# Attention set-up: 64 powers scanned and the rest made by ScalarE, chunk 0 scaled behind the reciprocal, a semaphore of its own for the gate, products of zeros first

## The chip, the cores and the metric

The kernel runs on one core of one Trainium2 chip. The metric is the device time of one execution in microseconds (us), here the median of three runs. The core's engines are TensorE (PE, with its weight loads as PEld), VectorE (DVE), ScalarE (ACT), GpSimd (POOL) and SyncE (SP), which issues most of the DMAs.

## The reference

Three stages follow one another. The change touches the set-up of the first one.

```python
# 1. linear attention with decay; B, H, S, D = 4, 8, 768, 48
for t in range(S):
    cur = einsum('bhd,bhe->bhde', u * k[t], v[t])
    y[t] = einsum('bhd,bhde->bhe', r[t], state + cur)
    state = w[:, :, None] * state + einsum('bhd,bhe->bhde', k[t], v[t])
# 2. top-1 mixture of experts on 3072 tokens of 384, 8 experts of 1024
x = gate_w[:, None] * (relu(x @ w1[e]) @ w2[e])        # e = argmax of the logits of a token
# 3. RMS norm and a gated feed-forward layer, 384 -> 1536 -> 384
out = (silu(xn @ w_gate) * (xn @ w_val)) @ w_out
```

## The kernel before

**The attention stage** cuts the 768 steps of each of 4 batches into 6 chunks of 128 (P); heads go in NP = 4 pairs, the two heads of a pair on partitions 0 to 47 and 64 to 111. In a chunk the recurrence becomes matrix products: queries are scaled by powers of the decay w and keys by inverse powers (rkt = rk_in * rk_decay, `scale_rk`, L795), TensorE makes the scores (`scores`, L1078), VectorE copies those below the diagonal into am, which already holds the bonus of u on its diagonal (L826, by the mask causal), and TensorE multiplies am by v (L1116) on top of what the state of the chunk before contributes (L1111). The next state needs kd = k * tail (POOL, L524), multiplied by v (L1103); tail is w raised to the remaining steps of the chunk. A last product turns y over and computes the logits in one go (`turn_x`, L1088, with turn_gate: the identity beside w_gate).

**Queues.** Each engine has its own program, whose instructions start in the order written, and they meet by semaphores. A chunk c (g counts chunks of all batches) is:
- VectorE (`batch`, L816): the two copies into am (L826), the bonus sum of chunk c + 1 (L802, needs POOL's ruk), `scale_rk` of chunk c + 2, the new state (L839), half of the diagonal of chunk c + 1 (L808), the sum of logits (L813). In chunk 2 of the first batch `token_setup` (L775) follows, which prepares what the routing needs.
- ScalarE (`batch`, L628): the decayed state (L635), x of the chunk before (L613, L614), the other half of the diagonal (L622), xt (L603).
- POOL (`batch`, L519): kd (L524), then ru = r * u (L514) and ruk = ru * k (L517) of the next chunk.
- TensorE (`batch`, L1091): scores of chunk c + 1, kd times v, `turn_x` of the chunk before, L1111, L1116.
- SP: load_columns (rk_in, three buffers; a load waits for `rk_scaled`), load_v, load_rows (rkn_in), and the stores of x.

**The set-up ahead of chunk 0.** VectorE scans w into powers 0 to 128 for each pair (L756); copies powers 0 to 63 to the upper half of r_decay (L758) and power 128 to chunk_decay (L759); takes the reciprocal of powers 64 down to 1 into its lower half (L761); copies r_decay in reverse into k_decay (L762); makes tail_t, the products of power 64 with powers 127 down to 0 (L766); then scales chunk 0 (L795); then `later_setup` waits for const_ld (L770), casts the mask to causal (L771), waits for the four memsets of POOL and raises z_ready; then bonus (L802) and half diagonal (L808) of chunk 0, and `scale_rk(0, 1)`. ScalarE issues the loads of u_b, const, turn_gate, bias_b, rms_gain and modality_i (L583 to L588), waits for const_ld, and copies the identity into turn_gate (L590). const_ld counts two loads, const (which holds the identity and the mask) and the gate's part of turn_gate. TensorE waits for const_ld (L1064), turns tail_t over (`decays_by_rows`, L1067), ScalarE copies that to tail (L596), and TensorE does the scores of chunk 0. POOL clears state and kd (L506), makes ru and ruk of chunk 0, and waits for tail before kd.

**Behind attention** the tokens are routed, the experts run in tiles of 256 tokens with weights and activations split in a high and a low part (three products each, L1156), and the feed-forward layer does the same in 6 blocks of 512 tokens.

## Time and profile before

| | |
|---|---|
| median of 3 runs | 861.05 us (860.03 to 861.21) |
| the profiled execution | 858.51 us |
| its span, first to last instruction | 856.7 us |
| mean granted TensorE clock | 0.98 of full |
| busy share of the span | PE 94%, DVE 41%, ACT 33%, POOL 18% |
| chain that ended last, by engine | PE 88%, DVE 6%, issue 2%, DMA 1%, ACT 1% |
| its largest line | L1156 (experts and feed-forward), 78% |
| bytes moved | 63.15 MB, mean 74 GB/s |

The attention stage is the first 139 us. The profile's page says where the whole time goes; of the first microseconds only the timeline, the chain of waits in order of time and the table of loads tell enough. Times in them count from the span's start. A row of the timeline merges equal instructions that follow one another: "x4" with 1.37 us are four instructions in 1.37 us. A matmul of fp32 operands leaves two records, so L1078's 8 matmuls count as 16. "DVEq" and the like are an engine's sequencer, "issue" a stretch in which it waited for nothing that the profile shows. In square brackets stands how long the engine had been idle and what ended that.

### The profile page before, as it was taken

What the parts mean: (1) busy time and instruction counts of PE and PEld (TensorE: products, weight loads), DVE (VectorE), ACT (ScalarE), POOL (GpSimd) and SP (SyncE); (2) the same over time, 40 slices, a digit from 0 to 9 for tenths busy, and PEclk for the clock granted to TensorE, in tenths of its full rate; (3) what the DMA queues carried; (4) which work ended last, traced back from release to release, by engine and by line L of the source; (5) the groups of instructions that cost most, each with busy time, mean ns of one, the idle gap of its engine ahead of it and who ended that gap; (6) DMA issues with size and microseconds to landing.
All of it is one profiled execution on the core that took longest, in us unless ns stands there. A gap on an engine that the chain in (4) does not pass through costs nothing.

```text
span 856.7 us, 14691 instructions
## 1 busy us (share of the span) xinstructions
PE 809.5 (94%) x5219; PEld 743.3 (87%) x5219; DVE 353.0 (41%) x662; ACT 285.6 (33%) x678; POOL 157.8 (18%) x138
## 2 busy tenths in 40 slices
PE   4999994499999999998999999999999999999998
PEld 4898883399999999997889888988988898898888
DVE  8999996643325332234252144024214402420330
ACT  3676672343335343333222123023212212221320
POOL 7787670312222122221000000000000000000000
PEclk9999998599999999999999999999999999999999
DMA  8688861421226222112000100110010001000001
GB/s 251 204 260 246 243 193 47 165 94 64 80 74 218 92 71 76 67 56 71 0 2 19 56 1 0 39 35 0 18 55 0 0 37 37 0 18 19 1 0 38
DMA packets 29034, 63.15 MB, mean 74 GB/s; under 512 B 4786, under 2 KB 17358, under 8 KB 28992
## 3 DMA queue, kind: packets, MB, share of 16 engines
q1 hardware_dynamic: 24224, 52.71, 19.4%
q0 software_dynamic: 3584, 9.46, 3.4%
q10 hardware_dynamic: 1184, 0.45, 0.2%
q8 instruction: 22, 0.36, 0.2%
q14 instruction: 20, 0.16, 0.1%
HBM read 49.62 MB, written 14.56 MB: 75 GB/s over the span
## 4 chain that ended last, share of the span: by engine, by line
PE 88%; DVE 6%; issue 2%; DMA 1%; ACT 1%; POOL 0%; DVEq 0%; ACTq 0%; POOLq 0%
PE bank L1156 78%; PE bank L1078 2%; PE bank L1116 2%; PE bank L1088 2%; PE bank L1103 1%; PE bank L1111 1%; PE bank L1149 1%; DVE am L808 1%; PE bank L1197 1%; DMA turn_gate<-w_gate 1%; DVE rkt L795 1%; DVE am L826 1%; DVE row_hot L915 1%; DVE bonus L802 1%; DVE state L839 1%
## 5 line engine op out<-in xcount | busy, mean ns | idle before, releaser
L1156 PE MATMUL bank<-xn_hi,ffn_hi 128*128 128x512 f32 x432 | 168.9, 391 | 2.9 <-DVE xn_lo L1022 2.9
L1156 PE MATMUL bank<-xn_lo,ffn_hi 128*128 128x512 f32 x432 | 168.7, 391 | 0.0
L1156 PE MATMUL bank<-xn_hi,ffn_lo 128*128 128x512 f32 x432 | 168.6, 390 | 0.0
L1041 DVE TENSOR_TENSOR prod<-silu,bank 128x512 f32<-128x512 f32 x72 | 49.5, 687 | 281.5 <-ACT silu L724 281.5
L724 ACT ACTIVATE silu<-bank 128x512 f32<-128x512 f32 x72 | 43.1, 598 | 221.2 <-PE bank L1156 221.2
L1156 PEld LDWEIGHTS bank<-xn_hi,ffn_hi 128*128 128x128 f32 x432 | 81.5, 189 | 19.9 <-issue 3.1
L1156 PE MATMUL bank<-ffn_hi,hh 128*128 128x384 f32 x288 | 97.1, 337 | 0.0
L1156 PE MATMUL bank<-ffn_hi,hl 128*128 128x384 f32 x288 | 96.3, 335 | 0.0
L1156 PE MATMUL bank<-ffn_lo,hh 128*128 128x384 f32 x288 | 96.3, 334 | 0.0
L1156 PEld LDWEIGHTS bank<-xn_hi,ffn_lo 128*128 128x128 f32 x432 | 81.5, 189 | 17.0
L1156 PEld LDWEIGHTS bank<-xn_lo,ffn_hi 128*128 128x128 f32 x432 | 81.5, 189 | 16.9
L1156 PE MATMUL bank<-xg_hi,w_hi 128*128 128x256 f32 x312 | 89.1, 286 | 2.0 <-DVE xg_lo L930 2.0
L1156 PE MATMUL bank<-xg_lo,w_hi 128*128 128x256 f32 x312 | 88.9, 285 | 0.0
L1156 PE MATMUL bank<-xg_hi,w_lo 128*128 128x256 f32 x312 | 88.9, 285 | 0.0
L968 DVE SCALAR_TENSOR_TENSOR h_lo<-bank,h_hi 128x512 fp32r<-128x512 f32 x52 | 35.9, 691 | 128.4 <-ACT h_hi L685 128.4
L1156 PE MATMUL bank<-w_hi,h_hi 128*128 128x384 f32 x208 | 71.0, 341 | 0.0
L1156 PE MATMUL bank<-w_hi,h_lo 128*128 128x384 f32 x208 | 69.9, 336 | 0.0
L1156 PE MATMUL bank<-w_lo,h_hi 128*128 128x384 f32 x208 | 69.9, 336 | 0.0
L1156 PEld LDWEIGHTS bank<-xg_hi,w_hi 128*128 128x128 f32 x312 | 60.5, 194 | 2.4 <-DVE xg_lo L930 2.4
L1156 PEld LDWEIGHTS bank<-xg_lo,w_hi 128*128 128x128 f32 x312 | 60.5, 194 | 0.0
L1156 PEld LDWEIGHTS bank<-xg_hi,w_lo 128*128 128x128 f32 x312 | 60.4, 194 | 0.0
L685 ACT ACTIVATE h_hi<-bank 128x512 fp32r<-128x512 f32 x52 | 31.1, 597 | 72.8 <-PE bank L1156 72.8
(146 smaller groups left out, 1247.7 us busy)
## 6 DMA issues: line engine op xcount, KB each, us to landing
rk_in<-rk_t SPq DMA_DIRECT2D x24, 448.0 KB, 4.3
rkn_in<-rk_n SPq DMA_DIRECT2D x24, 384.0 KB, 4.7
ffn_raw<-ffn_w SPq DMA_DIRECT2D x12, 576.0 KB, 3.7
w_raw<-w SPq DMA_DIRECT2D x16, 384.0 KB, 4.6
y_in<-y_tok SPq DMA_DIRECT2D x6, 770.0 KB, 4.5
v_in<-v_n SPq DMA_DIRECT2D x24, 192.0 KB, 4.2
x_tok<-x_sb SPq DMA_DIRECT2D x24, 192.0 KB, 2.3
out<-o_sb SPq DMA_DIRECT2D x24, 192.0 KB, 1.8
```

The costliest lines, as they stand in the source:

```text
L685: nc.scalar.activation(h_hi[:, FPQ * q:FPQ * q + FPQ, :], ps_h[q], ACT.Relu).then_inc(h_high, 1)
L724: nc.scalar.activation(silu[f % 2][:], ps_g[f % 2], ACT.Silu).then_inc(silu_ready, 1)
L795: v.tensor_tensor(rkt[c % IN][:], rk_in[c % IN][:], rk_decay[:], ALU.mult).then_inc(rk_scaled, 1)
L802: v.tensor_reduce(bonus[:], ruk[p][:], AX_X, ALU.add).then_inc(bonus_ready, 1)
L808: v.tensor_tensor(am[p][:, 0], ident.unsqueeze(1).to_broadcast([P, NP, P]), bonus[:, :, 0:1].to_broadcast([P, NP, P]), ALU.mult).then_inc( ...
L826: v.copy_predicated(am[p][:, q], causal[:], ps_a[p][q]).then_inc(a_ready, 1)
L968: v.scalar_tensor_tensor(h_lo[:, hq, :], ps_h[q], 0.0, h_hi[:, hq, :].bitcast(F32), ALU.max, ALU.subtract).then_inc(h_split, 1)
L1041: v.tensor_tensor(prod[f % 2][:], silu[f % 2][:], ps_v[f % 2], ALU.mult).then_inc(prod_ready, 1)
L1078: last = pe.matmul(ps_a[p][i][:, a, :], rkt[c % IN][rows, 1, a, :], rkt[c % IN][rows, 0, a, :], start=True, stop=True)
L1088: last = pe.matmul(ps_x[:, a, :], xt[p][:, a, :], turn_gate[:, a, :], start=True, stop=True)
L1116: last = pe.matmul(ps_y(a)[HALF * i2:HALF * i2 + D], v_in[i][:, a, i2, :], am[p][:, i2, a, :], start=False, stop=True, skip_group_check=True)
L1156: last = pe.matmul(dst, left[a], right[b2], start=first and n == 0, stop=end and n == 2)
```

## The change

- VectorE scans only powers 1 to 64. ScalarE makes powers 65 to 128 by scaling powers 1 to 64 with power 64, makes the copies into k_decay and r_decay, tail_t (four scaled copies in place of one product), causal and chunk_decay. The lower half of r_decay is still the reciprocal on VectorE; ScalarE copies it into k_decay behind it.
- VectorE scales chunk 0 as soon as that copy is done, then chunk 1 (before: behind the bonus and the half diagonal of chunk 0), then waits for const, sums the bonus, makes the half diagonal, waits for the memsets, raises z_ready, and waits for causal.
- The gate's load counts on a semaphore of its own, gate_ld, which TensorE waits for behind the scores of chunk 0 and the transposes; the waits for const_ld ask for const alone.
- The loads of bias_b, rms_gain and modality_i are issued behind ScalarE's part of the set-up.
- TensorE begins with 9 products of zeros (112 x 112 by 256 columns of fp32, from the cleared state[0] into bank 7, whose contents nobody reads), then does the scores of chunk 0 and after them the transposes of tail_t (before: the other way round).

```diff
@@ scalar
-            act.dma_start(turn_gate[:, :, PR:XW], w_gate).then_inc(const_ld, 16)
+            act.dma_start(turn_gate[:, :, PR:XW], w_gate).then_inc(gate_ld, 16)
+
+            act.wait_ge(powers_ready, 1)
+            nc.scalar.activation(k_decay[:, :, 0:MID], powers[:, :, MID - 1::-1], ACT.Copy)
+            nc.scalar.activation(r_decay[:, :, MID:P], powers[:, :, 0:MID], ACT.Copy)
+            for a in range(NP):
+                last = nc.scalar.activation(powers[:, a, MID + 1:P + 1], powers[:, a, 1:MID + 1], ACT.Copy,
+                                            scale=powers[:, a, MID:MID + 1])
+            last.then_inc(powers_all, 1)
+            act.wait_ge(inverse_ready, 1)
+            nc.scalar.activation(k_decay[:, :, MID:P], r_decay[:, :, MID - 1::-1], ACT.Copy).then_inc(decays_ready, 1)
+
+            act.wait_ge(powers_all, 1)
+            for a in range(NP):
+                last = nc.scalar.activation(tail_t[:, a], powers[:, a, P - 1::-1], ACT.Copy, scale=powers[:, a, MID:MID + 1])
+            last.then_inc(tail_t_ready, 1)
+            act.wait_ge(const_ld, 16)
+            nc.scalar.activation(causal[:], causal_f.unsqueeze(1).to_broadcast([P, NP, P]), ACT.Copy).then_inc(causal_ready, 1)
+            nc.scalar.activation(chunk_decay[:], powers[:, :, P], ACT.Copy)
+            nc.scalar.activation(turn_gate[:, :, 0:PR], ident[0:PR, 0:PR].unsqueeze(1).to_broadcast([PR, NP, PR]),
+                                 ACT.Copy).then_inc(products_ready, 1)
             for dst, src in ((bias_b, bias), (rms_gain, rms_g)):
                 act.dma_start(dst[:], src).then_inc(token_ld, 16)
             act.dma_start(modality_i[:].rearrange("p t w -> p (t w)"), modality.bitcast(I32)).then_inc(token_ld, 16)
-            act.wait_ge(const_ld, 16 * 2)
-            nc.scalar.activation(turn_gate[:, :, 0:PR], ident[0:PR, 0:PR].unsqueeze(1).to_broadcast([PR, NP, PR]),
-                                 ACT.Copy).then_inc(products_ready, 1)
...
-            act.wait_ge(const_ld, 16 * 2)
+            act.wait_ge(products_ready, 1)
             half_diagonal(0, 0)
@@ vector
-                wb = w_c[:, a:a + 1].to_broadcast([PR, P])
-                last = v.tensor_tensor_scan(powers[:, a, 1:P + 1], wb, wb, 1.0, ALU.mult, ALU.bypass)
-            link(last)
-            v.tensor_copy(r_decay[:, :, MID:P], powers[:, :, 0:MID])
-            v.tensor_copy(chunk_decay[:], powers[:, :, P])
-
-            link(v.reciprocal(r_decay[:, :, 0:MID], powers[:, :, MID:0:-1]))
-            v.tensor_copy(k_decay, r_decay[:, :, ::-1]).then_inc(decays_ready, 1)
+                wb = w_c[:, a:a + 1].to_broadcast([PR, MID])
+                last = v.tensor_tensor_scan(powers[:, a, 1:MID + 1], wb, wb, 1.0, ALU.mult, ALU.bypass)
+            last.then_inc(powers_ready, 1)
+            dve.wait_ge(powers_ready, 1)
+            v.reciprocal(r_decay[:, :, 0:MID], powers[:, :, MID:0:-1]).then_inc(inverse_ready, 1)
+            dve.wait_ge(inverse_ready, 1)
             dve.wait_ge(decays_ready, 1)
-            v.tensor_tensor(tail_t[:], powers[:, :, P - 1::-1], powers[:, :, MID:MID + 1].to_broadcast([PR, NP, P]),
-                            ALU.mult).then_inc(tail_t_ready, 1)
-
-            def later_setup():
-                dve.wait_ge(const_ld, 16 * 2)
-                link(v.tensor_copy(causal[:], causal_f.unsqueeze(1).to_broadcast([P, NP, P])))
-                dve.wait_ge(zeros, 4)
-                dve.sem_inc(z_ready, 1)
...
             scale_rk(0, 0)
-            later_setup()
+            scale_rk(0, 1)
+            dve.wait_ge(const_ld, 16)
             sum_bonus(0, 0)
             half_diagonal(0, 0)
-            scale_rk(0, 1)
+            dve.wait_ge(zeros, 4)
+            dve.sem_inc(z_ready, 1)
+            dve.wait_ge(causal_ready, 1)
             rounds(dve, batch, B)
@@ tensor (WARM = 9)
-                pe.wait_ge(const_ld, 16 * 2)
+                pe.wait_ge(const_ld, 16)
...
+            def zero_products(n):
+                for _ in range(n):
+                    pe.matmul(bank[7][0:PR, 0:2 * P], zero[:, 0:PR], zero, start=True, stop=True)
+
+            pe.wait_ge(zeros, 1)
+            zero = state[0][:, 0:2].rearrange("p a i d -> p (a i d)")
+            zero_products(WARM)
+            scores(0, 0)
             decays_by_rows()
-            scores(0, 0)
             pe.wait_ge(products_ready, 1)
+            pe.wait_ge(gate_ld, 16)
             pe.wait_ge(tail_ready, 1)
```

## Rows read from the trace of the kernel before

**Rows 1.** Chain that ended last, from the start: start us, us, what
```profile
1.67 7.83 DMA turn_gate<-w_gate
...
9.52 1.08 DVE causal L771
...
14.12 2.08 PE bank L1078 x16
...
36.02 1.91 PE bank L1116 x16
...
42.53 1.01 PE bank L1116 x16
```

**Rows 2.** Timeline of set-up: start us, us, engine line op out<-in [idle before]
```profile
2.43 0.66 ACTq L587 DMA_DIRECT2D bias_b<-bias  x1
...
2.89 1.37 DVE L756 TENSOR_TENSOR_SCAN powers<-w_c 112x128 f32<-112x128 f32 x4 [2.02 <-DMA w_c<-w_col]
...
3.60 0.45 ACTq L588 DMA_DIRECT2D modality_i<-modality  x1
...
4.58 1.75 DVE L761 RECIPROCAL rk_decay<-powers 112x256 f32<-112x256 f32 x1
...
6.96 1.41 POOL L514 TENSOR_TENSOR ru<-rkn_in,u_b 128x384 f32<-128x384 f32 x1 [4.32 <-DMA rkn_in<-rk_n]
7.43 2.02 DVE L795 TENSOR_TENSOR rkt<-rk_in,rk_decay 112x1024 f32<-112x1024 f32 x1
8.44 1.86 POOL L517 TENSOR_TENSOR ruk<-ru,rkn_in 128x384 f32<-128x384 f32 x1
...
9.54 1.01 PE L1067 MATMUL bank<-const,tail_t 112*128 112x112 f32 x4 [9.54 <-DMA turn_gate<-w_gate]
...
10.59 0.68 ACT L596 ACTIVATE tail<-bank 128x96 f32<-128x96 f32 x4 [0.49 <-PE bank L1067]
...
11.35 1.55 POOL L524 TENSOR_TENSOR kd<-rkn_in,tail 128x384 f32<-128x384 f32 x1 [1.04 <-ACT tail L596]
```

**Rows 3.** ScalarE by line and form to 30 us: xcount | busy us, mean ns
```profile
L622 ACT ACTIVATE am<-const,bonus 128x128 f32<-128x128 f32 x16 | 5.1, 399 | 2.8 <-DVE bonus L802 2.7
...
L603 ACT ACTIVATE xt<-bank 112x256 f32<-112x256 f32 x4 | 1.3, 381 | 2.8 <-PE bank L1116 2.7
...
L590 ACT ACTIVATE turn_gate<-const 112x448 f32<-112x448 f32 x1 | 0.6, 578 | 4.2 <-DMA turn_gate<-w_gate 4.2
```

**Rows 4.** Loads issued at 1.18, 2.58 and 3.23 us; last, us to landing
```profile
rk_in<-rk_t SPq DMA_DIRECT2D x1, 448.0 KB, 4.4
...
rk_in<-rk_t SPq DMA_DIRECT2D x1, 448.0 KB, 6.8
...
rkn_in<-rk_n SPq DMA_DIRECT2D x1, 384.0 KB, 7.4
```

**Rows 5.** By tile (rk_in, rkn_in), to 30 us: ns min/median/max
```profile
L795 DVE TENSOR_TENSOR rkt<-rk_in,rk_decay x5: 1202/1986/2019, 7.4 to 27.1; 112x1024 f32<-112x1024 f32 x5
...
L514 POOL TENSOR_TENSOR ru<-rkn_in,u_b x5: 1002/1409/1983, 7.0 to 26.2; 128x384 f32<-128x384 f32 x5
```

**Rows 6.** Timeline, VectorE and TensorE in the first chunks
```profile
15.95 0.55 DVE L802 TENSOR_REDUCE bonus<-ruk 128x8 f32<-128x384 f32 x1 [0.71 <-POOL ruk L517]
...
17.73 1.69 PE L1111 MATMUL bank<-rkt,state 112*112 112x128 f32 x8
...
19.35 1.08 PE L1116 MATMUL bank<-am,v_in 128*48 128x128 f32 x16
19.60 1.34 DVE L826 COPY_PREDICATED am<-causal,bank 128x512 f32<-128x512 uint8 x2 [0.18 <-DVE am L808]
...
25.34 1.35 DVE L826 COPY_PREDICATED am<-causal,bank 128x512 f32<-128x512 uint8 x2 [0.53 <-ACT am L622]
```

**Rows 7.** Timeline behind token_setup
```profile
34.63 1.33 DVE L826 COPY_PREDICATED am<-causal,bank 128x512 f32<-128x512 uint8 x2 [0.18 <-DVE bias_t L789]
```

**Rows 8.** Stretches: us, busy PE, PEld, DVE, ACT, POOL, granted clock, DMA
```profile
36.00:37.00 1.00, 0.98 (x10) 0.98 (x12) 1.00 (x2) 0.57 (x2) 0.00 (x0) 0.55 0.06 22
```

More of the change, by code:

```diff
@@ L46 @@
 IN = 3
+WARM = 9
 E, F = 8, 1024
@@ L332, in build @@
         const_ld = sem("const_ld")
+        gate_ld = sem("gate_ld")
         token_ld = sem("token_ld")
@@ L336, in build @@
         chain = sem("chain")
+        powers_ready = sem("powers_ready")
+        powers_all = sem("powers_all")
+        inverse_ready = sem("inverse_ready")
         decays_ready = sem("decays_ready")
+        causal_ready = sem("causal_ready")
         tail_t_ready = sem("tail_t_ready")
```

## The prediction

> **What bounds the kernel now.** I read the chain of waits first, since the change touches only the first microseconds and the question is what sets the end there. The chain starts at the load of turn_gate, issued at 1.67 us and landed 7.83 us later; L771 on VectorE, the bonus and the second scaling follow, and TensorE's scores of chunk 1 begin at 14.12 us [rows 1]. All this waits for a load that only the turning matmul and the logits need: L770 asks for both loads of const_ld. The timeline of set-up says what each engine does meanwhile [rows 2], and the timeline of the first chunks what holds it afterwards [rows 6]. Chunk 0 to chunk 3 are not bound by TensorE: at 34.63 us the copy into am of chunk 3 starts 0.18 us after the last step of token_setup on VectorE [rows 7], and TensorE, which is done before that, resumes at 36.02 us [rows 1]. So what counts up to 36 us is how early VectorE gets through its four chunks and token_setup. Behind 36.02 us the same loop runs on, and the matrix-heavy stages follow; the change alters none of that, so a shift at 36.02 us is a shift of the end, but for the clock.
>
> **Part by part: VectorE's head.** The first four scans of 128 take 1.37 us from 2.89 us [rows 2]. Halved in length they cost between 0.69 us (all of it by length) and 1.37; I take 0.8, powers ready at 3.7. The copies L758 and L759 leave VectorE, so the reciprocal (1.75 us [rows 2], same size) runs 3.75 to 5.5. ScalarE meanwhile makes two copies of 256 and four scaled ones of 64: its nearest rows are 0.33 us for each of a row of copies of 256 (1.3 us for four) and 0.32 for scaled ones of 128 (5.1 us for sixteen) [rows 3], so 0.66 + 4 x 0.24..0.32 = 1.6 to 1.9 us, done by 5.4 to 5.7, about when the reciprocal is. The last copy, 0.38 us [rows 3], ends at 5.95 to 6.1. rk_in of chunk 0 lands at 1.18 + 4.4 = 5.6 us [rows 4] and is no hindrance. The first scaling starts at 6.0, not 7.43 [rows 2].
>
> **The second scaling moved up.** rkt takes 2.02 us beside a POOL product, 1.20 without one [rows 2, 5]. Begun at 6.0, before rkn_in lands (6.96, where ru starts [rows 2]), it costs 1.2: done at 7.2; ru and ruk then have POOL's 1.0 each [rows 5] and end at 9.2, not 10.3. VectorE now stands in scale_rk(0, 1) until rk_in of chunk 1 lands: 2.58 + 6.8 = 9.4 us [rows 4]. Queued behind that wait are the bonus, both halves of the diagonal and the copy into am of chunk 0. It runs 9.4 to 10.6; bonus 0.55 [rows 6] to 11.15; ScalarE's four diagonals, 1.28, to 12.5; the copy, 1.34 [rows 6], to 13.85. Before, these steps were done about 1.4 us later.
>
> **tail and POOL.** ScalarE now has in its queue, ahead of tail: tail_t (4 x 0.32), causal (512 wide; nearest 0.58 for 448 [rows 3], so 0.65), chunk_decay (small, 0.1), turn_gate (0.58), and then the three DMA issues that used to stand ahead of the wait, 2.43 to 4.05 = 1.6 us [rows 2]. From 6.0 that is 7.3, 7.95, 8.05, 8.6, 10.2. The products of zeros start when the first memset is done, about 1.3 us. A matmul leaves two records; at the half clock eight of 128 columns take 1.69 us [rows 6], 0.21 each, so 0.42 for 256 columns and 18 x 0.42 = 7.6 us if the clock stays low, to 8.9; the clock was up by 19.35 us, where L1116 takes 1.08 us [rows 6], after work that ran on from 14.12 [rows 1], about 5 us, and if it does so again the products end near 7.5. Then come the scores of chunk 0, 2.08 us at half clock [rows 1] or about 1.1, and the transposes, 1.01 [rows 2] or half: ready at 9.2 to 10.6, at or just before ScalarE comes free. tail, 0.68 [rows 2], ends at 10.9; kd of chunk 0 starts at 11.0, not 11.35 [rows 2]. Behind it POOL has ru and ruk of chunk 1 (rkn_in lands at 3.23 + 7.4 = 10.6 [rows 4], no wait): three products of 1.0, plus 0.3 for VectorE's diagonal in between, to 14.35. Before, that was 15.95, where the bonus of chunk 1 sat 0.71 us for ruk [rows 6]. VectorE is free from 13.85, so this wait is still the last: **-1.6 us**.
>
> POOL's lock: the scaling's 2.02 against 1.20 [rows 2, 5] is what an exclusive turn looks like. The Trainium skill (SBUF — State Buffer, Who interferes with whom) says that whichever started first keeps the shared port for its whole instruction. By it kd, first at 11.0, would keep its 1.0 and the diagonal behind it would cost ru of chunk 1 its 0.6: ruk at 14.6 and 1.35 us gained here.
>
> **From bonus of chunk 1 on** the steps are those of before: 3.65 us to the copy at 19.60 [rows 6], now 18.0. The next copy, at 25.34, waited 0.53 us for ScalarE's diagonals [rows 6], which stand in its queue behind a turn that TensorE, late and at half clock until about 19 us, did late too. TensorE now gets to its chunk 1 about 3 us earlier, so the wait goes; what is late next is the usual 0.18 us between steps: **-0.35 us**. token_setup's loads land about 9 us after an issue that ends at 10.2, at 19, and are wanted at 28: nothing. The smaller steps that leave VectorE (L759, L762, L766, L771) are in these times already. The wait on causal_ready is met at 8.0: nothing. The gate's own semaphore is waited for by TensorE behind the transposes; landed at 9.5 [rows 1], nothing.
>
> **The clock.** TensorE stood 2 us before 36.02, and the granted clock was 0.55 from 36 to 37, near the lower of the two levels [rows 8]; L1116 took 1.91 us there, 1.01 once it was at 2.4 GHz [rows 1]. With the scores behind it, 2.08 us when all at half clock [rows 1] and about half that else, the low stretch cost some 1.7 us. Now VectorE is 2 us earlier at that point and TensorE 3, so the stand is about 3 us. The stretch behind it may be the same length (0) or hold one more group at half speed (+0.9, that same pair of rows); below nothing if it fails to come (-1.7). I take **+0.2**. The Trainium skill (TensorE: Matmul & The Clock Gate, Why this matters for your kernels) warns that an idle stretch between bursts brings the half clock back; by it a longer stand makes the fall certain and earlier, with the full +0.9, and the sum would be -1.05, or 860.0. Here the trace agrees in that the clock did fall.
>
> **Sum.** -1.6 - 0.35 + 0.2 = -1.75 us. The profiled execution took 858.51 us for a span of 856.7; it would take 856.8. The median of the timed runs is 2.5 us above the profiled one and takes the same difference: 861.05 - 1.75 = **859.3**.
>
> **Rivals.** (1) The half-clock stretch behind token_setup does not come, or its twin before the experts is shorter: for it speaks that a stand of 2 us is short, and may only just have brought the fall; against it that the stand grows. It gives -1.95 - 1.7: about 857.4. (2) The products of zeros don't raise the clock: they end at 8.9, scores and transposes at half clock at 12.0, tail at 12.75, kd at 12.85, ruk of chunk 1 at 16.2, 0.25 later than before; with the other terms (-0.35, +0.2) about 861.2. For it: between 9.5 and 19 us TensorE was at work and yet at half clock for most of the time. Against: that work had gaps. (3) The other side: the products hold TensorE. If they run no better than the four transposes did, 1.01 us for 4 x 112 columns [rows 2], a record of 256 costs 0.58 us and eighteen end at 11.7; kd then starts at 15.6, ruk of chunk 1 comes at 18.95, 3.0 us later: 863.9. It turns a loss above 0.2% from 0.52 us a record on; against it stands L1111's 0.21 for 128. (4) The change doesn't do what it says: ScalarE's part ends after the reciprocal by more than 0.5 us, or rk_in of chunk 1 lands later than 9.9, as its 6.8 us may, since VectorE now stands behind it. Each 1 us beyond costs 1 us; the gain is gone with 1.9: 861.0.
>
> **Chances.** Forecast 0.58, (1) 0.13, (2) 0.12, (3) 0.07, (4) 0.05, anything else on the slow side 0.05. About 0.2%, 1.7 us, is what a measurement of this kernel can tell from no change. The forecast lies at this edge: its own spread (0.35 us from the scans, 0.3 from the lock, 0.9 from the clock) puts a little over half of its chance beyond. So faster 0.32 + 0.13 = 0.45, same 0.26 + 0.17 = 0.43, slower 0.12. The range takes in the forecast's bounds, (1) and (2), and half a microsecond of the timed runs' spread: 857.0 to 861.6.
>
> **What would show it.** In the profile after: first scaling at 6.0 and second at 9.4; ruk of chunk 0 ending near 9.2; products of zeros ending before 8; kd of chunk 0 at 11.0; bonus of chunk 1 at 14.35; the copies into am at 18.0, 23.4 and, behind token_setup, 32.7; TensorE resuming at 34.1, at half clock. The prediction is wrong if kd of chunk 0 starts later than 12.6, if VectorE's copy behind token_setup stays at 34 or later, or if TensorE stays at half clock past 39.

## The result, and the profile after

Medians of five runs of each kernel: 860.03 us before (858.73 to 861.21), **854.52 us after** (853.33 to 857.50). The ratio is 0.9939 [0.9917, 0.9962], so 5.2 us less, [3.3, 7.1]. Forecast was 859.3 with a range of 857.0 to 861.6: the direction was right, the size was not, and the time lies below the range. The forecast was worked out from a median of 861.05 us for before, and this comparison has 860.03: with that base it would read 858.3, and the gain is still three times the 1.75 us forecast. The profiled execution of after was the slowest of its five (857.50 us, span 855.7), that of before a quick one (858.51 us, span 856.7), so the two traces are only 1.0 us apart; what the trace shows at the start is therefore looked at in two executions of after, this one and that of run a1, whose span was 849.6 us.

The head of the page of after, with the line of the granted clock:

```profile
span 855.7 us, 14738 instructions
...
PEclk8899998599999999999999999999999999999999
...
PE 89%; DVE 6%; issue 2%; DMA 1%; ACT 1%; POOL 0%; SPq 0%; DVEq 0%; POOLq 0%; ACTq 0%
PE bank L1179 78%; PE bank L1092 2%; PE bank L1102 2%; PE bank L1117 2%; PE bank L1130 2%; PE bank L1125 1%; PE bank L1172 1%; DMA rk_in<-rk_t 1%; DVE am L819 1%; PE bank L1220 1%; DVE am L837 1%; DVE rkt L806 1%; DVE row_hot L929 1%; DVE state L850 1%; DVE bonus L813 0%
```

The gate's load has left the chain; the second load of rk_in is in it now. The chain of after from the start (start us, us, what), to be held against [rows 1]:

```profile
2.58 8.39 DMA rk_in<-rk_t
10.96 0.02 issue
10.99 1.34 DVE rkt L806
12.33 0.14 issue
12.46 1.97 PE bank L1092 x16
```

Set-up in the timeline of after, to be held against [rows 2] (start us, us, engine line op out<-in [idle before]):

```profile
1.30 6.34 PE L1137 MATMUL bank<-state 112*112 112x256 f32 x18 [1.30 <-POOL state L512]
...
2.42 1.28 ACT L594 ACT_TABLE_LOAD   x1 [2.28 <-issue]
...
5.67 0.34 ACTq L613 DMA_DIRECT2D bias_b<-bias  x1
5.97 0.39 ACT L605 ACTIVATE tail_t<-powers 112x128 f32<-112x128 f32 x1
6.05 0.60 ACTq L613 DMA_DIRECT2D rms_gain<-rms_g  x1
6.16 1.23 DVE L806 TENSOR_TENSOR rkt<-rk_in,rk_decay 112x1024 f32<-112x1024 f32 x1 [0.55 <-ACT rk_decay L601]
...
7.58 1.16 PE L1092 MATMUL bank<-rkt 48*128 48x128 f32 x16
...
8.22 0.99 POOL L520 TENSOR_TENSOR ru<-rkn_in,u_b 128x384 f32<-128x384 f32 x1 [5.59 <-DMA rkn_in<-rk_n]
...
9.31 0.68 ACT L619 ACTIVATE tail<-bank 128x96 f32<-128x96 f32 x4 [0.99 <-PE bank L1081]
10.24 0.99 POOL L530 TENSOR_TENSOR kd<-rkn_in,tail 128x384 f32<-128x384 f32 x1
10.99 1.33 DVE L806 TENSOR_TENSOR rkt<-rk_in,rk_decay 112x1024 f32<-112x1024 f32 x1 [3.61 <-DMA rk_in<-rk_t]
...
12.46 1.97 PE L1092 MATMUL bank<-rkt 48*128 48x128 f32 x16 [3.19 <-DVE rkt L806]
...
34.34 1.33 DVE L837 COPY_PREDICATED am<-causal,bank 128x512 f32<-128x512 uint8 x2 [0.17 <-DVE bias_t L800]
...
35.72 1.23 PE L1130 MATMUL bank<-am,v_in 128*48 128x128 f32 x16 [2.52 <-DVE am L837]
```

Two things are to be seen. The products of zeros end at 7.64 us and raised the clock: the scores of chunk 0 take 1.16 us, where [rows 1] had 2.08. But in this execution the load of rk_in for chunk 1 landed late, VectorE stood 3.61 us for it and TensorE 3.19, and the scores of chunk 1 were back at 1.97 us, half clock. So TensorE resumes at 35.72, only 0.30 us earlier than the 36.02 of before.

The same stretch in the second execution of after (a1, the fastest of its six) shows how far the start can come forward when the load lands as forecast:

```profile
9.04 1.27 DVE L806 TENSOR_TENSOR rkt<-rk_in,rk_decay 112x1024 f32<-112x1024 f32 x1 [1.73 <-DMA rk_in<-rk_t]
...
10.16 1.02 POOL L530 TENSOR_TENSOR kd<-rkn_in,tail 128x384 f32<-128x384 f32 x1 [0.92 <-ACT tail L619]
...
10.46 1.16 PE L1092 MATMUL bank<-rkt 48*128 48x128 f32 x16 [1.09 <-DVE rkt L806]
...
13.71 0.55 DVE L813 TENSOR_REDUCE bonus<-ruk 128x8 f32<-128x384 f32 x1
...
31.80 1.33 DVE L837 COPY_PREDICATED am<-causal,bank 128x512 f32<-128x512 uint8 x2 [0.17 <-DVE bias_t L800]
...
33.19 1.88 PE L1130 MATMUL bank<-am,v_in 128*48 128x128 f32 x16 [3.40 <-DVE am L837]
```

**Where the time went, by stage.** Five points of the trace that every kernel has: TensorE's resumption behind token_setup; VectorE's `chosen`, the first step behind attention; TensorE's first transposes for the experts (they wait for the gather); its first feed-forward product; the end of the span. Times in us:

| kernel | resumes | chosen | transposes | feed-forward | end |
|---|---|---|---|---|---|
| before | 36.02 | 141.30 | 162.56 | 401.38 | 856.7 |
| after | 35.72 | 143.00 | 164.18 | 401.96 | 855.7 |
| after, second execution (a1) | 33.19 | 137.30 | 158.42 | 395.91 | 849.6 |

From before to after's own trace: -0.30 at the start, +2.00 in the rest of attention, -0.08 in the routing, **-1.04 in the experts and -1.58 from the first feed-forward product on**, sum -1.0. To the second execution: -2.83, -1.17, -0.14, **-1.33, -1.6**, sum -7.1. Some 2.6 to 2.9 us come from stages that the change does not touch. The first two columns scatter: the two executions of the same kernel differ by 2.5 us where TensorE resumes and by 5.7 us at `chosen`, so no single pair of traces prices the start.

**The place.** Between the last expert product and the first feed-forward product ScalarE squares and copies the last tokens and then makes xn_hi. Timeline of ScalarE, before:

```profile
397.37 0.48 ACT L705 ACTIVATE y_sb<-bank 128x384 f32<-128x384 f32 x1
399.77 1.84 ACT L711 ACTIVATE xn_hi<-bank,rms_gain 128x512 fp32r<-128x512 f32 x3 [1.91 <-issue]
```

and after:

```profile
399.96 0.48 ACT L728 ACTIVATE y_sb<-bank 128x384 f32<-128x384 f32 x1
400.34 1.85 ACT L734 ACTIVATE xn_hi<-bank,rms_gain 128x512 fp32r<-128x512 f32 x3
```

Before, ScalarE stood 1.91 us, and the profile names nothing that it waited for. After, the same instruction follows at once. Between the two instructions ScalarE's program leaves the nested `If` blocks of the expert tiles (`over_tiles`, L300 to L312 of before), so it jumps there, over the code of tiles that are not needed. TensorE's timeline says what that does to its first feed-forward product. Before:

```profile
401.38 0.76 PE L1156 MATMUL bank<-xn_hi,ffn_hi 128*128 128x512 f32 x1 [2.88 <-DVE xn_lo L1022]
```

After:

```profile
401.96 0.47 PE L1179 MATMUL bank<-xn_hi,ffn_hi 128*128 128x512 f32 x1 [0.88 <-DVE xn_lo L1036]
```

TensorE stood 2.88 us in the one and 0.88 in the other, and the product itself takes 0.76 us against 0.47. The chain of before has the stand and the stretch behind it (start us, us, what):

```profile
398.52 1.25 issue
399.77 0.69 ACT xn_hi L711
400.49 0.76 DVE xn_lo L1022
401.38 50.80 PE bank L1156 x216
```

and that of after:

```profile
401.96 49.23 PE bank L1179 x216
```

The first 216 feed-forward products take 50.80 us in the one, 49.23 in the other. The rows of stretches of before name the reason (columns as in [rows 8]):

```profile
402.00:404.00 2.00, 2.00 (x6) 1.60 (x5) 0.55 (x1) 0.91 (x1) 0.00 (x0) 0.50 0.54 109
```

and of after:

```profile
402.00:404.00 2.00, 2.00 (x9) 1.66 (x10) 1.13 (x2) 1.47 (x2) 0.28 (x1) 1.00 0.05 8
```

Behind the stand of 2.88 us TensorE's clock is at the lower level for 3.4 us (0.50 in this stretch); behind that of 0.88 it stays up (1.00). My reading of the chain of before ended at 60 us, and took in neither row.

### The profile page after: what moved, and what is told of

The parts are those of the page before. It is cut to its first block, busy times and chain, and to the rows that moved or that the text cites. A ratio compares the mean times of both kernels' runs of the same rounds, so it can differ in the third digit from the quotient of the medians.

```text
span 855.7 us, 14738 instructions
## 1 busy us (share of the span) xinstructions
PE 816.0 (95%) x5237; PEld 748.3 (87%) x5237; DVE 349.3 (41%) x657; ACT 289.2 (34%) x691; POOL 152.7 (18%) x138
## 4 chain that ended last, share of the span: by engine, by line
PE 89%; DVE 6%; issue 2%; DMA 1%; ACT 1%; POOL 0%; SPq 0%; DVEq 0%; POOLq 0%; ACTq 0%
PE bank L1179 78%; PE bank L1092 2%; PE bank L1102 2%; PE bank L1117 2%; PE bank L1130 2%; PE bank L1125 1%; PE bank L1172 1%; DMA rk_in<-rk_t 1%; DVE am L819 1%; PE bank L1220 1%; DVE am L837 1%; DVE rkt L806 1%; DVE row_hot L929 1%; DVE state L850 1%; DVE bonus L813 0%
```

## The experiments

The first question is whether the stand of ScalarE belongs to the change at all. The theory: it comes from where ScalarE's later instructions lie in its program, which the change moved by 13 activations and some waits; the rival: it follows from the order of the work at the start. The second question is which parts of the start bring the rest. Ratios are to the kernel before on the same chip. No kernel leaves any of the reference's work out.

**a1: the changed kernel once more**, unaltered.

> The changed kernel once more, for a second trace. What moved the median by 5.5 us is open. Theory A: the gain has two parts, the start (about 2 us until TensorE resumes behind token_setup) and the step from the experts to the feed-forward layer, where ScalarE waited 1.91 us for nothing the profile shows before xn_hi in the kernel before and not in the one after; with the half clock that follows such a stand it is 3.6 us. Then xn_hi starts again right behind y_sb here, the first product of the feed-forward layer comes 2.5 us after the last one of the experts (4.5 before), and the ratio is 0.993 to 0.995. Theory B: the loads' landing and the clock vary by chance from run to run; then this trace shows the stand before xn_hi as likely as not, and the ratio may be 0.997 or more.

0.9930 [0.9908, 0.9952], median 853.94 beside 860.46. The gain is real and its size is 4 to 8 us, as the first of the two expectations had it. Its trace is shown above: no stand ahead of xn_hi.

**a2: after without the products of zeros.**

```diff
-WARM = 9
+WARM = 0
```

> The changed kernel without the nine products of zeros. If they matter only through the clock in the first two chunks (theory A, and the prediction), TensorE has slack there, the stand behind token_setup is set by VectorE, and the time is that of the changed kernel within 0.5 us. If they are the cause of the gain (rival: the clock's later stretches hang on them), it goes back towards the time before by 2 us or more.

0.9950 [0.9934, 0.9967], against 0.9930 and 0.9939 for after with zeros. TensorE's matmuls are at half speed until about 18 us (L1117's eight records take 1.81 us at 13.44, and 1.02 at 19.30). By these ratios the zeros are worth 0.9 to 1.7 us, between the two expectations (within 0.5 us, or 2 us and more), but the intervals overlap.

**a3: before with the products of zeros.**

```diff
+            pe.wait_ge(zeros, 1)
+            zero = state[0][:, 0:2].rearrange("p a i d -> p (a i d)")
+            for _ in range(9):
+                pe.matmul(bank[7][0:PR, 0:2 * P], zero[:, 0:PR], zero, start=True, stop=True)
             decays_by_rows()
```

> The kernel before with only the nine products of zeros put ahead of TensorE's first work. ScalarE's program is that of before, so by theory A xn_hi behind the experts again waits about 1.9 us for nothing shown, and the time is that of before within 0.7 us (the scores of chunk 0 and 1 at full clock save at most 0.9 us each, of which VectorE hides most). If the products are the cause: 2 us or more faster.

0.9991 [0.9973, 1.0009]: nothing, as expected. The transposes ran at full speed (0.60 us for 1.01), but they start at 10.03, when the gate's load has landed, and VectorE's second scaling stands behind that same load. My reading is that the zeros pay only where TensorE is what is waited for. This run does not show it alone: in its trace TensorE stood 2.40 us ahead of the scores of chunk 1, and from 14.6 to 18.1 us the granted clock was down again, so part of what the zeros brought was lost there. The stand of 1.69 us ahead of xn_hi is there, as in before.

**a4: before, with ScalarE's program lengthened.** Sixteen increments of a semaphore that nobody reads, between attention and the experts, where ScalarE waits anyway.

```diff
+            spare = sem("spare")
+            for _ in range(16):
+                act.sem_inc(spare, 1)
             act.wait_ge(experts_ready, 1)
```

> The kernel before with 16 semaphore increments that nobody waits for, in ScalarE's program between attention and the experts, where ScalarE stands for 10 us anyway. They only move ScalarE's later code by about as many instructions as the change does. Theory A in the form that the stand before xn_hi is ScalarE fetching its code: the stand goes, and with it 2.0 us, or 3.6 with the half clock behind it: ratio 0.996 to 0.998. If it is chance or something of the data: ratio 1.000 and the stand of 1.9 us stays.

0.9966 [0.9953, 0.9978]: **2.9 us less than before, from sixteen instructions that do nothing** (expected 0.996 to 0.998 if the stand goes). The timeline of ScalarE in this kernel:

```profile
398.89 0.48 ACT L708 ACTIVATE y_sb<-bank 128x384 f32<-128x384 f32 x1
399.26 1.85 ACT L714 ACTIVATE xn_hi<-bank,rms_gain 128x512 fp32r<-128x512 f32 x3
```

The stand is gone, and the first 216 feed-forward products take 49.26 us. The start is that of before (TensorE resumes at 36.62). So the stand does not come from the order at the start.

This trace shows one more thing, which the rows of before could not. VectorE's tail_t in before, and then in this one:

```profile
6.82 0.69 DVE L766 TENSOR_TENSOR tail_t<-powers 112x512 f32<-112x512 f32 x1
...
7.02 1.50 DVE L769 TENSOR_TENSOR tail_t<-powers 112x512 f32<-112x512 f32 x1
```

In before it began ahead of POOL's ru (6.96) and took 0.69 us. Here, 0.2 us later, ru was already on (6.98) and tail_t took 1.50, so that the first scaling started at 8.43 us, not at 7.43. The traces of d1 to d4 have 1.36 to 1.52 and a first scaling at 8.23 to 8.32; of the seven with the old set-up only before and a3 have the short one. The changed set-up, which has no tail_t on VectorE, starts its first scaling at 6.08 to 6.38 in all its traces but c2's. The forecast took the quick case for the rule.

**c1: after without zeros and with the old order of TensorE's first two steps.**

```diff
-WARM = 9
+WARM = 0
...
-            scores(0, 0)
             decays_by_rows()
+            scores(0, 0)
```

> The changed kernel without products of zeros, and with the transposes of tail_t ahead of the scores of chunk 0 again. Without the products alone the time was 856.43 us (853.94 with them), and kd of chunk 0 began at 11.26 us instead of 10.16, because scores and transposes ran at half clock one behind the other. Theory A (what the products give is kd earlier): tail_t is ready at 7.2, the transposes end at 8.3, kd begins near 9.2, and the time is that of the changed kernel, 854 us, ratio 0.993. Theory B (they give by the clock: TensorE late in chunks 0 and 1): kd is early but the time stays near 856.4, ratio 0.995.

0.9953 [0.9936, 0.9969], the second of the two expectations. kd of chunk 0 starts at 9.35 us, 0.8 earlier than in a1, and it brings nothing over a2: TensorE at half clock is late with everything that follows, and the copy into am of chunk 2 waits for ScalarE's diagonals again:

```profile
23.92 1.35 DVE L837 COPY_PREDICATED am<-causal,bank 128x512 f32<-128x512 uint8 x2 [0.58 <-ACT am L645]
```

That is the 0.53 us of [rows 6]. What the zeros bring is then the clock and not the order, as far as intervals tell that also overlap with those of after.

**c2: after with the three small loads issued ahead of ScalarE's work.**

```diff
             act.dma_start(turn_gate[:, :, PR:XW], w_gate).then_inc(gate_ld, 16)
+            for dst, src in ((bias_b, bias), (rms_gain, rms_g)):
+                act.dma_start(dst[:], src).then_inc(token_ld, 16)
+            act.dma_start(modality_i[:].rearrange("p t w -> p (t w)"), modality.bitcast(I32)).then_inc(token_ld, 16)
             act.wait_ge(powers_ready, 1)
```

(and removed from behind turn_gate's copy.)

> The changed kernel with the loads of bias_b, rms_gain and modality_i issued ahead of ScalarE's set-up, as before. ScalarE's first copies then wait for 1.6 us of issues and the table load behind them (start 5.3 instead of 3.9 us), the first scaling starts at 7.6 instead of 6.1, kd of chunk 0 about 1.4 us later. If the start is bound by this chain: 1 to 1.5 us slower than the changed kernel (ratio 0.9945 to 0.995 to before). If it is bound by the landing of rk_in of chunk 1, which VectorE waits for until 9.0 to 11.0: within 0.5 us.

0.9966 [0.9951, 0.9980], that is 2 to 3 us worse than after, where 1 to 1.5 was expected; the rest is not explained (its trace has 10.2 us of low clock behind token_setup, where after has 6.8 and a1 3.4). The table load of ScalarE starts when the issues ahead of it are through:

```profile
3.07 0.45 ACTq L594 DMA_DIRECT2D rms_gain<-rms_g  x1
3.55 0.46 ACTq L595 DMA_DIRECT2D modality_i<-modality  x1
4.04 1.28 ACT L598 ACT_TABLE_LOAD   x1 [3.90 <-issue]
7.41 1.88 DVE L807 TENSOR_TENSOR rkt<-rk_in,rk_decay 112x1024 f32<-112x1024 f32 x1 [1.80 <-ACT rk_decay L605]
```

4.04 for 2.42, and the first scaling starts at 7.41 for 6.16. Ahead of the first activation a DMA issue costs its full time (1.62 us for three); behind queued activations it costs nothing, as the rows of after above show: the issues at 5.67, 6.05 and 6.68 run while ScalarE makes its last copy of the decays and tail_t, although the program has them behind the copy into turn_gate, which starts at 7.76.

**c3: after with the second scaling in its old place**, behind the half diagonal of chunk 0.

```diff
             scale_rk(0, 0)
-            scale_rk(0, 1)
...
             dve.sem_inc(z_ready, 1)
+            scale_rk(0, 1)
```

> The changed kernel with the scaling of chunk 1 behind the bonus and half diagonal of chunk 0 again. In the changed kernel VectorE stands 1.7 to 3.6 us at this scaling for rk_in while ruk of chunk 0 is ready. If that stand is on the path: bonus of chunk 0 at about 9.3 us, the copy into am of chunk 0 near 11.8, up to 1 us faster than the changed kernel. If POOL's ruk of chunk 1 holds the next step anyway: the same within 0.5 us.

0.9941 [0.9923, 0.9960]: the same as after within the intervals, the second of the two expectations. Its trace resumes at 34.26, between the two of after. Moving the scaling up neither gained nor cost anything that these intervals can tell (about 2 us).

**c4: after with token_setup moved** to the last chunk of the last batch.

```diff
+                    if isinstance(b, int) and b == B - 1 and c == NC - 1:
+                        token_setup()
                     if c or not first:
                         sum_logits(g - 1, 1 - p)
-                    if first and c == 2:
-                        token_setup()
```

> The changed kernel with token_setup moved from chunk 2 to the last chunk of the last batch, ahead of its sum of logits, where VectorE stands for 3.6 us. Nothing else changes. If the stand behind token_setup and the half clock that follows cost what the traces show (TensorE stands 2 to 3.4 us, then 3.4 to 6.8 us at half clock, 1.7 to 3.4 lost), TensorE runs on at full clock from 20 to 130 us and the time is 3 to 5 us less, less up to 1.2 for what of the 4.8 us does not fit in the gap at the end: 850 to 851.5 us. If VectorE is the real bound of the attention stage, its 4.8 us come back as waits later in it, and the time stays within 1 us of 854.

**0.9872 [0.9854, 0.9890], median 849.11: faster than both kernels.** The expected gain on after was 3 to 5 us, less up to 1.2; it is 5.4. TensorE's stand at 33 us and the half clock behind it are gone. Stretches of this kernel:

```profile
33.00:37.00 4.00, 4.00 (x50) 3.56 (x49) 3.90 (x9) 2.45 (x9) 3.92 (x4) 1.00 0.78 232
...
20.00:60.00 40.00, 39.62 (x465) 35.79 (x466) 38.88 (x66) 29.43 (x106) 36.97 (x27) 1.00 0.85 263
```

beside those of after:

```profile
20.00:60.00 40.00, 37.14 (x400) 33.57 (x399) 36.40 (x63) 25.02 (x92) 28.22 (x23) 0.91 0.72 215
```

The copy into am of chunk 3 starts at 27.24 us, 4.6 before that of a1, and `chosen` comes at 133.69, 3.6 before: token_setup now runs where VectorE has more room, at the end of attention.

**d1 and d2: before with 4 and with 64 of the idle increments** (the diff of a4 with another count).

> The kernel before with 4 instead of 16 idle semaphore increments in ScalarE's program ahead of the experts (16 gave a ratio of 0.9966 and no stand before xn_hi). Theory A, code that is or is not there yet depending on where it lies: the trace shows either the stand of 1.7 to 1.9 us and a ratio of 1.000, or no stand and 0.9966; never something between. The rival (the increments help in another way, by delaying or ordering something): no stand and a smaller gain in proportion.

> The same with 64 increments, some 3 us of ScalarE's stand of 10 us. Theory A: again one of the two, with the stand and 1.000, or without it and 0.9966. If the stand is gone for 4, 16 and 64, the kernel before merely lies in a narrow bad place.

1.0003 [0.9992, 1.0014] and 0.9996 [0.9981, 1.0011]: no gain, and nothing in between, as theory A had it. The stand is there in both, and in both the profile gives it to another releaser than in before (1.91 us in d1, 1.66 in d2). ScalarE in d1:

```profile
402.43 1.84 ACT L714 ACTIVATE xn_hi<-bank,rms_gain 128x512 fp32r<-128x512 f32 x3 [1.91 <-PE bank L1200]
```

L1200 is not what held it: the 12 transposes of that line end at 401.54, 0.89 us before xn_hi starts, and in a4 xn_hi starts while they still run (398.47 to 400.00). So it is not that more instructions help more: sixteen do, and 0, 4 or 64 do not, a matter of position.

**d3: a4 with the gate's load on its own semaphore.** One part of the change on the padded kernel, free of the stand.

```diff
-            act.dma_start(turn_gate[:, :, PR:XW], w_gate).then_inc(const_ld, 16)
+            act.dma_start(turn_gate[:, :, PR:XW], w_gate).then_inc(gate_ld, 16)
...
-                dve.wait_ge(const_ld, 16 * 2)
+                dve.wait_ge(const_ld, 16)
...
             pe.wait_ge(products_ready, 1)
+            pe.wait_ge(gate_ld, 16)
```

> The kernel before with the 16 increments (0.9966 without more) and, of the change, only the gate's load on a semaphore of its own. const lands at 5.8 us, the gate at 9.5 or later, so transposes and tail come early and kd of chunk 0 starts behind ruk at 10.3 instead of 11.4 to 12.2; bonus of chunk 1 comes 1 us earlier. If the shared semaphore was most of the start's loss: ratio 0.995 to 0.9955, that is, half or more of what the whole rewritten set-up gives (0.993 to 0.994). If VectorE's set-up is: 0.9966, no change.

0.9964 [0.9951, 0.9978], a4's own ratio and the second of the two expectations. kd of chunk 0 starts at 10.32 instead of 12.24 and the bonus of chunk 1 at 15.22 instead of 16.35, but the copy of chunk 2 starts at 25.99 against 25.80:

```profile
25.99 1.35 DVE L830 COPY_PREDICATED am<-causal,bank 128x512 f32<-128x512 uint8 x2 [0.91 <-ACT am L623]
```

The 1.1 us were given back while TensorE worked at half clock. The load that headed the chain of waits of before was worth nothing on its own that the intervals (0.0013 to each side) can tell.

**d4: a4 with the late token_setup** (both diffs above).

> The kernel before with the 16 increments and token_setup in the last chunk of the last batch; nothing of the change. On the changed kernel the move gave about 5 us (0.9872 against 0.9935). If that is a stand and a half-clock stretch common to both: ratio 0.990 to 0.9915. If it only pays because the new set-up is early: 0.995 or more.

0.9908 [0.9889, 0.9927], 0.58% or 5.0 us below a4, inside the first expectation. On after the same move brought 0.9935 to 0.9872 (0.9935: mean of its two ratios), 5.4 us. It does not need the change.

**e1: after with 48 idle increments**, to bring the stand back.

> The changed kernel with 48 idle semaphore increments in ScalarE's program ahead of the experts. The kernel before has the stand ahead of xn_hi with 0, 4 and 64 increments and not with 16; the change adds 13 instructions and some waits to ScalarE, about as many as the 16. If place alone decides, 48 more bring the changed kernel to where 64 brought the one before: the stand of 1.7 to 1.9 us is back, with half clock behind it, and the ratio is 0.996 to 0.997 instead of 0.9935. If the change removes the stand in another way: no stand, 0.993 to 0.994.

0.9980 [0.9967, 0.9993], median 858.12 beside 860.29. The stand is back as expected; the ratio lies above the 0.996 to 0.997 forecast for that case, so the start is worth less or the stand costs more than I then thought:

```profile
396.42 0.48 ACT L731 ACTIVATE y_sb<-bank 128x384 f32<-128x384 f32 x1
398.80 1.84 ACT L737 ACTIVATE xn_hi<-bank,rms_gain 128x512 fp32r<-128x512 f32 x3 [1.89 <-issue]
```

The 216 products take 50.82 us. **With the stand on both sides the change is worth 0.20%, 1.7 us [0.6, 2.8].** Against after itself (0.9935) the stand costs 0.45%, 3.9 us.

**e2: c4 without the products of zeros** (WARM = 0).

> The changed kernel with the late token_setup (0.9872), without the nine products of zeros. Behind the set-up there is then neither a stand nor a low stretch that could hide or double what the products do. If the products are worth the 1.5 to 2 us that the runs with and without them show (0.9935 against 0.9950): ratio 0.989 to 0.9895. If that difference was the later clock's chance: 0.987 to 0.988.

0.9885 [0.9866, 0.9904] against 0.9872 [0.9854, 0.9890]: 1.1 us for the zeros, between the two expectations and again with overlapping intervals. In both pairs (after against a2, c4 against e2) the zeros come out about 1 us or more ahead; that is likely, not settled.

**All sixteen traces together.** The executions with the stand (before, a3, d1, d2, e1) and those without (after, a1, a2, a4, c1, c2, c3, c4, d3, d4, e2) do not overlap in two stretches. From the experts' transposes to the first feed-forward product it is 238.56 to 239.19 us, mean 238.87, with it, and 236.90 to 238.40, mean 237.71, without; the 216 products behind (taken whole in the chain of before, after, a1, a2, a3, a4, c1, c2, c3, d1 to d4, e1 and e2) are 50.77 to 50.85 against 49.21 to 49.26. That is 1.16 + 1.56 = 2.7 us, beside the 2.9 that a4's ratio gives.

**What the same traces say of the start.** Four executions have the old set-up and order with nothing else changed in attention (before, d1, d2, a4), three the new one with its zeros (after, a1, e1). Means, in us:

| | copy into am behind token_setup | TensorE resumes | chosen |
|---|---|---|---|
| old set-up | 35.18 | 36.56 | 142.82 |
| new set-up | 33.21 | 34.59 | 140.07 |
| difference | -1.97 | -1.97 | -2.74 |

Within each group `chosen` spreads over 2.7 and 5.7 us, so these are rough; they lie between the 1.7 us of e1 and the 3.1 of a1 against a4.

**What moves in the memory traffic at the stand.** The table of DMA queues lists two of the kind "instruction" (q8 and q14), by that name code of the engines, in pieces of 16 and 8 KB. In all sixteen traces one piece of each starts where ScalarE passes from the experts to xn_hi. In the five with the stand the 8 KB piece starts within 0.25 us of the stand's beginning, and xn_hi starts 1.33 to 1.38 us after that piece has landed, in every one of them; the end of the 16 KB piece lies 0.16 to 0.83 us ahead of it. In the eleven without, the same two pieces start -0.11 to +0.29 us from xn_hi's own start, and it comes without a stand.

## Why the prediction was wrong, step by step

**The step that failed** is the sentence that the change alters nothing of the later stages, "so a shift at 36.02 us is a shift of the end, but for the clock". It holds for what is computed, not for where the instructions lie. ScalarE's new position took away a stand of 1.9 us at 398 us and 3.4 us of half clock behind it. That is 2.7 us by the traces, 2.9 by a4 and 3.9 by e1, half or more of a result of 5.2. The prediction put this term at nothing, without a row for it. The row for it was in the trace of before: the "issue" of 1.25 us at 398.52 is by far the longest such piece of the chain behind 300 us, and of ScalarE's own idle times behind set-up 1.9 us for xn_hi is the only one above 0.3 put down to "issue".

**The sum for the start, -1.75 us, was about right, perhaps short.** e1, which has the stand on both sides, gives -1.7 [-2.8, -0.6]. Without the stand on either side (a1 against a4, 0.9930 to 0.9966) it is -3.1 us, of which the interval allows 1.75 too. At the copy behind token_setup the mean of the traces is -1.97 where the forecast has -1.95. That it comes out so is in part luck: the terms were wrong in both directions, and the old set-up was read in its quick case (first scaling at 7.43 us; 8.23 to 8.43 in five of seven traces). Two of the three signs of being wrong that the prediction named did come in after's own profile: the copy behind token_setup is at 34.34, and the clock is low until 43.4 us. In a1 neither did (31.80, and low until 36.7). The terms by themselves, from a1's trace, which is of the fastest execution:

- *First scaling at 6.0, second at 9.4*: 6.08 and 9.04. ruk of chunk 0 done at 9.2: 9.24. Zeros done by 8: 7.74. Right.
- *ScalarE is held 1.6 us by three DMA issues, kd at 11.0*: wrong. They ran beside its activations, ScalarE was free at 8.24 and stood 1.17 us for the transposes; kd started at 10.16. I had charged a sequencer's time to the engine. The term -1.6 for ruk of chunk 1 therefore became -2.24 for its bonus (13.71 for 15.95), and TensorE became what tail waits for, so that zeros and clock can weigh more than I gave them.
- *Copies at 18.0, 23.4 and 32.7*: 17.30, 22.57 and 31.80, so -2.83 at the last, for the -1.95 of the sum; but 34.34 in after and 33.48 in e1. The wait for ScalarE's diagonals of chunk 2, -0.35, went as said in a1; in c1 and d3, with TensorE at half clock, it stayed (0.58 and 0.91).
- *TensorE resumes at 34.1 at half clock*: 33.19, at half clock, so L1130 takes 1.88 us.
- *rk_in of chunk 1 lands at 9.4*: the term with the widest scatter. VectorE's second scaling, which waits for it, started at 8.98 (c4), 9.04 (a1), 9.73 (c1), 9.89 (c2), 10.02 (a2), 10.25 (e1), 10.74 (e2) and 10.99 (after). The fourth rival priced 1 us for each us beyond 9.9; after's trace bears out the direction and adds half clock to it: 1.95 us later than a1 at the scaling, 2.53 later where TensorE resumes. Before did not depend on it, since its second scaling came at 11.96.
- *Clock behind token_setup, +0.2*: a length cannot be forecast to that. TensorE stood 2.52 us in after and 3.40 in a1; the low stretch was 6.8 us in after, 3.4 in a1. Before had 3.4 behind its 2.06 us, a2 3.4 behind 2.76, a4 6.8 behind 2.21, d1 10.2 behind 2.59. The 3.4 us that after has more than before are worth about half of that, 1.7 us (an estimate from the two levels of the clock), most of the +2.00 in the rest of attention.

**The rivals.** (1), no half clock: did not come, in no trace with token_setup in its old place. (2) and (3), zeros that raise nothing or hold TensorE: fell; in the seven traces with zeros the 18 records took 5.90 to 7.34 us, 0.33 to 0.41 each, and the scores of chunk 0 ran at 1.16 in all of them. (4), a late rk_in: came in the profiled execution, at 10.99. That the time would come out below 857 I had tied to the clock alone.

**The two rules of the Trainium skill.** On POOL's lock (SBUF — State Buffer, Who interferes with whom): the first scaling took 1.23 us alone for the 2.02 of [rows 2], and in after ru and ruk 0.99 each with no VectorE beside them, as an exclusive turn would have it; tail_t ahead of ru or behind it (0.69 and 1.50 us, under a4) is the same thing. The toll that I put on ru of chunk 1 came too: in a1 it took 1.45 us at 11.14, with VectorE's half diagonal on until 11.73. The 0.25 us less gain that I drew from it can't be told from the other terms. On the clock (TensorE: Matmul & The Clock Gate, Why this matters for your kernels): an idle stretch between bursts did bring half clock back, behind token_setup (2.52 and 3.40 us idle) and in after already at 12.46, behind 3.19 us. So far the traces agree with the rule. The length of the idle stretch did not settle it here: the clock fell behind 2.06 us in before and at 11.8 us in c4, behind 1.41, and did not fall behind 1.09 in a1 and 1.92 in c3 (12.00 us). Its +0.9 for a longer stand came in after, as 3.4 us more of low clock than before, and not in a1.

**What stays open.** That the engine waits at the stand for its own code is my reading: no semaphore is late, 0, 4 and 64 increments have it while 16 do not, ScalarE's program jumps there, and in all five traces xn_hi starts the same 1.33 to 1.38 us behind a transfer of that queue. The queue does not say whose code that is, and no run takes the jump away, so it is supported and not shown. That after and before differ by 5.2 us where the start gives 1.7 to 3.1 and the stand 2.7 to 3.9 is an account that closes within the intervals, not a proof of each part.

## What to carry to other kernels

Follow the chain of waits to the end of the span before you say that a change at the start alters nothing behind it, and price each "issue" in it: a stand with no releaser on an engine whose program is about to get longer or shorter can vanish or appear, and runs of the old kernel padded with idle instructions, at more than one count (4 and 64 showed nothing, 16 did), tell how much of a difference is that. Read the old kernel from more than one trace: two engines that reach the same step within 0.2 us of each other can swap, here for 1.0 us at the first scaling. Charge a DMA issue to the engine only if no earlier work is queued on it. And before shortening a set-up, look for the one block of work that stalls the critical engine in mid-stage: moving token_setup was worth 5.0 and 5.4 us on the two kernels, where the new set-up itself brought 1.7 to 3.1.

## What the runs showed of the hardware that was not expected

- ScalarE stood 1.66 to 1.91 us ahead of one instruction behind a jump, depending on the length of its program before it: on before with 0, 4 or 64 extra instructions and on after with 48, but not on before with 16 or on after as it is. With the half clock that follows it cost 2.7 to 3.9 us. In the five traces that have it the instruction started 1.33 to 1.38 us after an 8 KB transfer of the queue of kind "instruction" had landed.
- The releaser printed for such a stand can be wrong: "issue" in before and e1, a bank of TensorE in d1 and d2.
- DMA issues on ScalarE's sequencer (0.34, 0.60 and 0.48 us) ran beside its activations; ahead of its first activation the same three (0.62, 0.45 and 0.46) pushed the table load from 2.42 to 4.04 us.
- The low stretch of TensorE's clock behind a stand of the same size, 3.40 us, was 3.4 us in a1, 6.8 in c3 and 10.2 in c2. Products of zeros had it at its higher level when the scores started at 7.6 us, instead of at about 18; idle stretches of 3.19 us (after) and 1.41 us (c4) took it down again, one of 1.92 us (c3) did not.
- VectorE's tail_t took 0.69 us when it began ahead of POOL's ru and 1.36 to 1.52 when it began behind it.
- The same load at the same place of the queue (448 KB, issued at 2.58 us) was waited for until 8.98 to 10.99 us in different executions.
